# The second weight transfer of a three-stage kernel is issued without waiting for the first values

## The reference, cut to what matters

```python
# attention: 4 batches x 8 heads x 768 rows x 64; chunks of 32 rows see 8 memory keys + 56 keys around them
scores = scale * np.matmul(q_c, k_full.transpose(0, 1, 3, 2))
scores = scores - np.max(scores, axis=-1, keepdims=True)
a = np.exp(scores)
a = a / (np.sum(a, axis=-1, keepdims=True) + 1e-09)
out[:, :, c_start:c_end] = np.matmul(a, v_full)
# first layer: x is 3072 x 512, w_in 512 x 2048, w_out 2048 x 512
h = x @ w_in
g = h * np.cos(h)
x = g @ w_out
# second layer: w1, w2, w3 512 x 768, w_out 768 x 512
h = np.maximum(np.maximum(x @ w1, x @ w2), x @ w3)
return h @ w_out
```

## Time and profile before

| | us |
|---|---|
| median of three runs | 1080.54 |
| the three runs | 1082.39, 1079.06, 1080.54 |
| span of the profiled execution | 1079.6 |
| PE busy | 1032.5 (96%) |
| PEld busy | 984.1 (91%) |
| DVE busy | 538.5 (50%) |
| ACT busy | 330.7 (31%) |
| POOL busy | 83.6 (8%) |

### The profile page before, as it was taken

One profiled execution on the slowest core, in us unless ns is written; L12 is line 12 of the kernel. 1 busy time (PEld: TensorE's weight loads), 2 busy tenths in 40 slices (PEclk: granted clock), 3 DMA queues, 4 the chain that ended last, 5 costly groups with the idle time before them and its releaser, 6 DMA issues.

```text
span 1079.6 us, 17509 instructions
## 1 busy us (share of the span) xinstructions
PE 1032.5 (96%) x6976; PEld 984.1 (91%) x6976; DVE 538.5 (50%) x1132; ACT 330.7 (31%) x575; POOL 83.6 (8%) x64
## 2 busy tenths in 40 slices
PE   5797999999999999999999977999999999999998
PEld 4687999999999999999999976999999999999997
DVE  5576665665665666665665666323222322233222
ACT  2455354344353353353443443101110101101000
POOL 1554000000000000000000354000000000000000
PEclk7699999999999999999999999999999999999999
DMA  8743231241321321311320231201010000000000
GB/s 212 183 143 117 69 89 40 52 107 30 73 77 40 89 49 42 101 39 40 89 59 11 70 97 59 85 4 59 3 58 30 29 29 29 29 29 29 0 30 30
DMA packets 35722, 66.05 MB, mean 61 GB/s; under 512 B 2368, under 2 KB 26944, under 8 KB 35648
## 3 DMA queue, kind: packets, MB, share of 16 engines
q1 hardware_dynamic: 31616, 50.34, 16.9%
q0 software_dynamic: 4032, 14.68, 4.2%
HBM read 52.43 MB, written 12.58 MB: 60 GB/s over the span
## 4 chain that ended last, share of the span: by engine, by line
PE 84%; DVE 8%; ACT 5%; DMA 2%; issue 1%; SPq 0%; ACTq 0%; DVEq 0%
PE ps L305 23%; PE ps L307 23%; PE ps L306 23%; DVE stage_and_tiles L662 3%; PE ps L461 3%; PE ps L462 3%; PE ps L460 3%; PE ps L350 2%; PE ps L324 2%; ACT wts L531 2%; DMA qk<-qk_in 1%; DVE stage_and_tiles L668 1%; ACT stage_and_tiles L506 1%; PE ps L358 1%; ACT stage_and_tiles L504 1%
## 5 line engine op out<-in xcount | busy, mean ns | idle before, releaser
L305 PE MATMUL ps<-xh,wts 128*128 128x384 f32 x1088 | 375.2, 345 | 3.1 <-issue 1.7
L307 PE MATMUL ps<-xh,wts 128*128 128x384 f32 x1088 | 366.6, 337 | 0.0
L306 PE MATMUL ps<-xl,wts 128*128 128x384 f32 x1088 | 365.9, 336 | 0.0
L305 PEld LDWEIGHTS ps<-xh,wts 128*128 128x128 f32 x1088 | 205.8, 189 | 14.7 <-issue 10.8
L306 PEld LDWEIGHTS ps<-xl,wts 128*128 128x128 f32 x1088 | 206.1, 189 | 2.0
L307 PEld LDWEIGHTS ps<-xh,wts 128*128 128x128 f32 x1088 | 205.7, 189 | 0.0
L305 PE MATMUL ps<-gh,wts 128*128 128x384 f32 x512 | 172.2, 336 | 13.1 <-DVE gl L680 12.8
L662 DVE TENSOR_SCALAR stage_and_tiles<-stage_and_tiles 128x384 f32<-128x384 f32 x128 | 76.6, 598 | 212.8 <-ACT stage_and_tiles L506 212.8
L307 PE MATMUL ps<-gh,wts 128*128 128x384 f32 x512 | 171.4, 335 | 0.0
L306 PE MATMUL ps<-gl,wts 128*128 128x384 f32 x512 | 171.1, 334 | 0.0
L512 ACT ACTIVATE stage_and_tiles<-stage_and_tiles,half_pi 128x384 f32<-128x384 f32 x128 | 79.0, 617 | 237.2 <-DVE stage_and_tiles L677 237.1
(11 more groups left out here) (63 smaller groups left out, 828.3 us busy)
## 6 DMA issues: line engine op xcount, KB each, us to landing
qk<-qk_in SPq DMA_DIRECT2D x46, 384.0 KB, 5.1
wraw<-w_in POOLq DMA_DIRECT2D x28, 512.0 KB, 3.7
vals<-v_in SPq DMA_DIRECT2D x46, 256.0 KB, 3.8
y_dram<-stage_and_tiles SPq DMA_DIRECT2D x8, 768.0 KB, 6.3
qk<-y_dram SPq DMA_DIRECT2D x8, 768.0 KB, 4.3
out<-stage_and_tiles SPq DMA_DIRECT2D x8, 768.0 KB, 3.6
stage_and_tiles<-qk_in SPq DMA_DIRECT2D x2, 384.0 KB, 9.2
stage_and_tiles<-v_in SPq DMA_DIRECT2D x2, 256.0 KB, 6.2
```

Source lines behind the costliest of these rows:

```text
L305: pe.matmul(o, wh, mh, start=start, stop=False)
L306: pe.matmul(o, wh, ml, start=False, stop=False)
L307: return pe.matmul(o, wl, mh, start=False, stop=stop)
```

## The change

POOL no longer waits for `v_landed` before it issues the transfer of slot 1.

```diff
             plan = [(w1_in, s) for s in range(NF)] + [(w2_in, s) for s in range(WSLOTS2)]
             load_w(*plan[0], 0)
-            pool.wait_ge(v_landed, 32)
             load_w(*plan[1], 1)
             for g in range(len(plan)):
                 low_w(plan[g][1], g)
```

## The result

| | before | after |
|---|---|---|
| median of 20 runs, us | 1081.88 | 1083.21 |
| range of the runs, us | 1079.06 to 1083.83 | 1081.81 to 1084.28 |
| span of the profiled execution, us | 1079.6 | 1080.1 |

The ratio is 1.0013, with a 95% interval of 1.0007 to 1.0018: the change costs 1.4 us (0.8 to 1.9, from the ratio times 1081.88). It is real and it is small.

What follows compares the result with a forecast made beforehand. Landing data bounds the start (20.0 of 33.6 us), PE is 98% busy from 106 us. Wait 0, moved issue 0, traffic ahead of piece 2 1.6 us: 1080.5 + 1.6 = 1082.1 us, range 1079.2 to 1084.6.

Steps and rivals of the forecast that it cites:

- The removed wait holds up nobody: On POOL before slot 1's transfer: removing the 12.70 us wait gains 0 us, since slot 1 lay ready 3.6 us early.
- 1.6 us of SP's queue: Slot 1's 512 KB pass ahead of piece 2 on full DMA engines, delaying it 1.6 us; bounds 0.6 and 2.2.
- Piece 1 near 14.2: PE's scores of piece 1 begin near 14.2 us and not at 12.56.
- Piece 2 near 19.9: PE's scores of piece 2 begin near 19.9 us and not at 18.25.
- Slot 2 meets the values as before, and their 5.24 us stay: Slot 2 and piece 2's values are issued later together, so the values' transfer still takes 5.24 us.
- The first layer matmul moves to about 35.2: At the end of the start, PE's first layer matmul moves from 33.62 to about 35.2 us.
- all that is left of the start is instruction time: After piece 2's values land, only instruction time remains, so the first layer matmul shifts from 33.62 to about 35.2.
- rival (c): In the start, later work meets PE's high clock earlier: gain 2.7 us minus 1.6, giving 1079.4 us; chance 0.10.
- There is no slack between start and end: From start to end, PE busy 98% from 106 to 1076.5 us, the 1.6 us comes through in full.
- The first block is a cycle of ACT and DVE of 5.73 us: After the start, the first block runs on ACT and DVE, one step in 5.73 us.
- Rival (a): The start doesn't move, as slot 1 already cost piece 2 as much at its end: 1080.5 us; chance 0.18.
- Rival (b): A low PE clock stretch falls on steps with 24 matmuls, 2.6 us more: 1084.7 us; chance 0.14.

Runs made afterwards that it cites:

- run 5: Changed kernel, but SP issues slot 1 on its own queue behind piece 2, with no wait of its own: 1081.24 us, ratio 0.9996.
- its repeat: The changed kernel measured again with no edit (numbered 1), beside the kernel before: 1084.03 us, ratio 1.0017.
- run 3: Kernel before, with POOL waiting for DVE's last clearing instead of the values before issuing slot 1: 1083.15 us, ratio 1.0010.
- run 6: Kernel before, with ACT casting slot 3 behind its first copy and angle: 1081.73 us, ratio 0.9999.
- run 8: Kernel before, with all casts of the first block behind that step's copy and angle: 1078.46 us, ratio 0.9976.
- run 9: run 8 plus the low parts of the first layer's 16 slots made by DVE instead of POOL: 1066.34 us, ratio 0.9854.
- run 7: Changed kernel, with ACT casting slot 3 behind its first copy and angle: 1083.60 us, ratio 1.0024.
- run 4: Changed kernel plus two useless POOL transfers of 256 KB right behind slot 1: 1085.14 us, ratio 1.0031.
- run 2: Kernel before, with POOL's wait before slot 1 moved from the values to the keys of piece 1: 1081.67 us, ratio 0.9994.
- run 10: run 6 plus slot 0 also held behind the first values and cast two operations later: 1079.59 us, ratio 0.9982.
- run 11: run 9 plus slots 0 and 1 both held behind the first values, slot 0 cast two operations later: 1065.02 us, ratio 0.9841.

## Why the prediction was right, step by step

- "The removed wait holds up nobody": right. POOL waited for ACT's cast in its place (16.28 us), and ACT cast slot 1 at 26.97, in its own order; the times of run 5 show no cost and no gain once the transfer is back behind piece 2.
- "1.6 us of SP's queue": right. Piece 2 moved by 1.12 us in the profile after, 1.68 in its repeat, 1.27 in run 3; the second 512 KB added 1.7 us by the times. The lower bound of 0.6 is excluded by the times (interval from 0.8 on), and so is the upper one of 2.2 by the first 20 runs, though not by the repeat. What slot 1 cost piece 2 in before, which the prediction used for its lower bound only (up to 1 us, "not proven by any row"), is there: SP's queue had 36.2% in 17:18, and up to 0.7 us comes back. With slot 1 in its old place piece 2 lands at 18.11, 17.95, 17.99 and 18.18 (before, runs 6, 8 and 9), with slot 1 at once at 19.24, 19.80 and 19.07 (after, runs 1 and 7): 1.3 us later on average, so this term measures about 1.3 and not 1.6.
- Piece 1 near 14.2: 13.62 and 14.21. Piece 2 near 19.9: 19.37 and 19.93. Piece 1 was said not to be on the chain, and in run 3 the loss is there without it.
- "Slot 2 meets the values as before, and their 5.24 us stay": nearly; 5.50 in the profile after.
- "The first layer matmul moves to about 35.2": wrong, 33.89 and 33.94. The step that failed is "all that is left of the start is instruction time". Those instructions run on PE's clock, and it was at 1.00 where before it had been at 0.50. This was rival (c)'s mechanism. That it could give back so little, because ACT was free only 0.1 us before PE was done (37.26 and 37.37), was luck for the number.
- "There is no slack between start and end": right in the sum, but for a reason that the prediction lacked. When PE is early, ACT stands before the landing of slot 3 (36.22 in the profile after, 37.43 in the repeat), and that path is late too, as it starts at the copy of piece 2. Behind it stands POOL's low part of slot 3, which holds DVE. In the profiled pair all this left 0.27 us at the second angle and 0.5 in the spans, in the repeat 1.44 at the second angle. That both paths carry the loss into the times is argued from these profiles and not shown; run 7 shows that it doesn't come only over slot 3's landing.
- "The first block is a cycle of ACT and DVE of 5.73 us": the number held (48.70, 54.46, 60.23 after), the description did not. POOL was in the cycle too: 1.4 us of each turn were DVE standing behind POOL's low part. For the change it counts once, in the first step, where the low part of slot 3 sets how late the cycle begins.
- Rival (a), no shift: excluded by the interval of the 20 runs. Rival (b), a worse clock: nothing of it in the profile after, where in 40:60 us the clock was 1.00 against 0.83 before. But it is in the repeat: in 108:114 us, near the end of the first block, the clock is 0.72, and from the angle at 108.92 to the end of the span are 973.7 us, where before it was 1.00, and 972.1 us from the angle at 107.47. Of the 3.0 us between those two spans (1082.6 and 1079.6) half comes from there.

Left open: which way the clock falls in one execution. Three profiles of the same early start (after, repeat, run 7) had different stretches at 0.50, and no run controlled it. The low stretch near the end of the first block is in four of five profiles with 512 KB or more ahead of piece 2 (runs 1, 3, 4 and 7, not after) and in two of five without (runs 2 and 10; not before, 5 and 6). That is too few to tell whether a later start brings it more often; if it does, part of the 1.4 us is clock. It would not explain that the time follows the bytes, -2.1 (run 10 against run 6), 0, 1.4 and 3.4 us. Also open is why piece 0 lands at 6.7 to 7.1 us in most profiles, at 7.7 and 8.8 in runs 9 and 8 and at 10.5 to 10.7 in runs 2 and 5; slot 0's packets are in flight then, but slot 0 was not taken away without other changes until runs 10 and 11, which are two profiles (scores at 6.99 and 7.25) and no proof.

## What to carry to other kernels

A wait in front of a transfer that is not needed soon may be the thing that keeps its bytes out of the way; before it is removed, look at whether the DMA engines are full at the time and whose landing stands on the chain, and price the bytes that pass ahead of that landing. If early issue is wanted, put the transfer on the queue behind the one that matters; in run 5 that cost nothing. And when an instruction takes four times what the same one takes elsewhere, look for what the neighbouring engine was doing in just that time: moving work from POOL to DVE, which was the busier of the two, was worth 15.8 us here together with the casts' new place, over ten times the change under study.

## What the runs showed of the hardware that was not expected

- A DVE instruction of 0.35 us (lines 662 and 674, which read `stage_and_tiles` and write it or `gh`) takes 1.8 to 2.5 us when it starts while POOL's subtraction of 128x1024 (2.4 to 2.6 us) is running, and it ends about 0.2 us after POOL's. Not every DVE instruction does: line 649, which reads one operand from `ps`, takes 0.69 us whether POOL subtracts (26.96 us in before) or not. DVE does POOL's subtraction in 1.22 us.
- POOL's transfers start moving late and then push SP's aside: 96.1% against 0.8% of the engines in 6:7 of the changed kernel, though two microseconds on both move (69.9% and 34.5% in 8:9). An issue at 8.15 moved its bytes only from 12 us, one at 14.01 only from 17, one at 15.09 from 17. For the one at 8.15 it was not DVE's clearing, which had ended, that held it: DVE was idle from 10.56 to 14.21.
- The granted clock in the profile after is given as 1.00 for 8 to 20 us, yet 32 scores matmuls take 1.93 us there, as they do at 0.50 before. That trace has no record of the clock before 24.6 us. Where the clock column and the matmuls' own pace differ at the start of a trace, the pace is to be believed:

```profile
8.00:14.00 6.00, 1.29 (x28) 0.86 (x23) 1.55 (x3) 0.63 (x1) 0.00 (x0) 1.00 1.07 248
...
13.62 1.94 PE L323 MATMUL ps<-stage_and_tiles 128*32 128x128 f32 x32 [4.71 <-DMA stage_and_tiles<-qk_in]
```
